# GpSimd's sums of weights on a new timetable, with the order of the first loads, of the pair products and of the parts of x, in a fused attention and matmul-chain kernel

## The reference

```python
scores = q @ k.T / sqrt(64)              # 4 batches, 8 heads, 576 positions, head size 64
scores = where(0 <= i - j < 64, scores, -1e9)
attn = exp(scores - max); attn = attn / (sum(attn) + 1e-9)
x = (attn @ v) as 2304 tokens x 512
x = ((x @ w1) * (x @ w2)) @ w3 @ w_out   # 512 -> 1024 -> 1024 -> 512
h = x @ w_in                             # 512 -> 2048
out = maximum(0.01 * h, h) @ moe2_w_out  # 2048 -> 512, 2304 x 512 out
```

## Time and profile before

| | |
|---|---|
| median of 3 runs | 741.69 us (739.91 to 742.8) |
| profiled execution | 744.82 us, span 742.9 us |
| granted TensorE clock, mean | 0.995 |
| PE (TensorE matmul) busy | 727.1 us, 98% |
| DVE busy | 530.3 us, 71% |
| ACT busy | 417.2 us, 56% |
| POOL busy | 93.3 us, 13%, all before slice 14 of 40 |
| transfers | 181.13 MB, mean 244 GB/s |

### The profile page before, as it was taken

How to read it: one execution, slowest core, us unless ns; L and a number is a source line. 1 busy time by engine, 2 the same in 40 slices (tenths; PEclk the granted TensorE clock), 3 DMA queues, 4 the chain that set the end, 5 groups by cost and what they waited for, 6 DMA issues and landing times.

```text
span 742.9 us, 13803 instructions
## 1 busy us (share of the span) xinstructions
PE 727.1 (98%) x5032; PEld 700.1 (94%) x5032; DVE 530.3 (71%) x833; ACT 417.2 (56%) x889; POOL 93.3 (13%) x122
## 2 busy tenths in 40 slices
PE   8999999799999999999999999999999999999998
PEld 7788898698989999999999999999999999999997
DVE  5988987569657867888867968658788755455552
ACT  5876576536655345656545656456678544444541
POOL 3433574203334000000000000000000000000000
PEclk9999999989999999999999999999999999999999
DMA  9885657645674289988857988988997568777773
GB/s 339 271 292 170 199 184 251 191 155 158 221 241 160 98 271 349 321 276 315 285 195 275 330 293 271 356 303 277 332 375 273 147 163 231 213 211 231 212 199 115
DMA packets 96835, 181.13 MB, mean 244 GB/s; under 512 B 7936, under 2 KB 55680, under 8 KB 96768
## 3 DMA queue, kind: packets, MB, share of 16 engines
q1 hardware_dynamic: 90032, 166.62, 68.4%
q10 hardware_dynamic: 6736, 13.63, 5.0%
HBM read 111.80 MB, written 68.42 MB: 243 GB/s over the span
## 4 chain that ended last, share of the span: by engine, by line
PE 77%; DMA 10%; DVE 6%; issue 2%; SPq 2%; POOL 2%; ACT 1%; DVEq 0%; ACTq 0%
PE acc L402 14%; PE acc L403 14%; PE acc L404 14%; PE ps_pair L403 5%; PE ps_pair L402 5%; PE ps_pair L404 5%; DMA raw_a<-wsum_between 4%; PE ps_more L402 3%; PE ps_values L402 3%; PE ps_more L403 3%; PE ps_values L403 3%; PE ps_more L404 3%; PE ps_values L404 3%; DMA weight_sums<-raw_a 2%; PE ps_values L1672 1%
## 5 line engine op out<-in xcount | busy, mean ns | idle before, releaser
L402 PE MATMUL acc<-parts,weights_a 128*128 128x384 f32 (+1 forms) x320 | 112.2, 351 | 1.9 <-DVE arena L1388 1.3
L402 PE MATMUL acc<-parts,weights_b 128*128 128x384 f32 x320 | 110.3, 345 | 0.9 <-DVE arena L1326 0.5
L404 PE MATMUL acc<-parts,weights_a 128*128 128x384 f32 (+1 forms) x320 | 109.5, 342 | 0.0
L403 PE MATMUL acc<-parts,weights_a 128*128 128x384 f32 (+1 forms) x320 | 109.3, 341 | 0.0
L404 PE MATMUL acc<-parts,weights_b 128*128 128x384 f32 x320 | 108.0, 338 | 0.0
L403 PE MATMUL acc<-parts,weights_b 128*128 128x384 f32 x320 | 108.0, 337 | 0.0
L1457 DVE TENSOR_TENSOR parts<-raw_c,parts 128x768 fp32r<-128x768 f32 x64 | 61.2, 958 | 62.1 <-ACT parts L955 62.0
L955 ACT ACTIVATE parts<-raw_c 128x768 fp32r<-128x768 f32 x64 | 54.0, 846 | 69.6 <-DMA raw_c<-g_between 65.9
L402 PEld LDWEIGHTS acc<-parts,weights_a 128*128 128x128 f32 x320 | 60.1, 188 | 6.8 <-issue 3.1
L402 PEld LDWEIGHTS acc<-parts,weights_b 128*128 128x128 f32 x320 | 60.9, 190 | 2.7 <-issue 0.8
L404 PEld LDWEIGHTS acc<-parts,weights_a 128*128 128x128 f32 x320 | 60.0, 188 | 1.8
(11 more groups left out here) (212 smaller groups left out, 1776.6 us busy)
## 6 DMA issues: line engine op xcount, KB each, us to landing
g_between<-arena SPq DMA_DIRECT2D x75, 384.0 KB, 4.8
raw_c<-g_between SPq DMA_DIRECT2D x64, 384.0 KB, 3.5
arena<-p_between SPq DMA_DIRECT2D x42, 384.0 KB, 5.1
arena<-qk_steps SPq DMA_DIRECT2D x36, 384.0 KB, 5.0
arena<-v_steps SPq DMA_DIRECT2D x36, 256.0 KB, 3.3
p_between<-arena SPq DMA_DIRECT2D x24, 384.0 KB, 5.2
x_between<-arena ACTq DMA_DIRECT2D x21, 384.0 KB, 5.2
arena<-x_between SPq DMA_DIRECT2D x21, 384.0 KB, 5.6
```

What stands on the lines that cost most here:

```text
L402: eng.matmul(out_ap, w_hi, m_hi, start=start, stop=False, skip_group_check=resumed)
L403: eng.matmul(out_ap, w_hi, m_lo, start=False, stop=False, skip_group_check=resumed)
L404: return eng.matmul(out_ap, w_lo, m_hi, start=False, stop=stop, skip_group_check=resumed)
```

## The change

`PRE_SLOT` is new: in the first eight halves twelve slots apart (nine where none of the attention's loads lies), in the last four seven; `load_pre(u+1)` stands four slots after `presums(u)` in place of three. v of steps 0 and 1 is loaded in slot 2, and the first two units of w1 and w2 in slots 1 and 2, in place of ahead of slot 0 and in slot 1. In each round `make_p22` moves up to the second P3 product, and `make_p12` moves behind `make_p21`. The parts of x are split with P3 ahead of P7, and t4 and P4's part later.

```diff
-XS_ORDER = (P2, P1, P5, P6, P7, P3, P4)
+XS_ORDER = (P2, P1, P5, P6, P3, P7, P4)
-PRE_SLOT = (21, 27, 33, 39, 50, 66, 72, 78, 84, 90, 96, 108)
+PRE_SLOT = (24, 36, 48, 57, 69, 81, 93, 105, 115, 122, 129, 136)
+P0_LOAD = {1: 0, 2: 1, 4: 2, 8: 3}
-XS_HI_FIRST = {2: P6, 4: P7, 5: P3, 6: P4}
+XS_HI_FIRST = {2: P6, 3: P3, 4: P7, 7: P4}
-XS_HI_NEXT = {1: P7, 2: P3, 4: P4}
-XS_LO_FIRST = {0: "t2", 1: "t3", 2: P6, 4: "t4", 5: P7, 7: P3, 8: P4}
+XS_HI_NEXT = {1: P3, 2: P7, 7: P4}
+XS_LO_FIRST = {0: "t2", 1: "t3", 2: P6, 4: P3, 5: P7, 6: "t4", 8: P4}
-XS_LO_NEXT = {-1: P6, 0: "t3", 2: P7, 3: "t4", 4: P3, 5: P4}
+XS_LO_NEXT = {-1: P6, 0: "t3", 3: P3, 4: P7, 5: "t4", 8: P4}
@@ SP, before and in the first 16 slots
-            load_v(0)
-            load_fill(0)
-            load_v(1)
-                if k in P0_SUMS and P0_SUMS[k] + 1 < HALF_UNITS:
-                    load_fill(P0_SUMS[k] + 1)
+                if k == 2:
+                    load_v(0)
+                    load_v(1)
+                if k in P0_LOAD:
+                    load_fill(P0_LOAD[k])
@@ SP, stage A/B
-                    if PRE_SLOT[u] + 3 == n and u + 1 < NPRE:
+                    if PRE_SLOT[u] + 4 == n and u + 1 < NPRE:
                         load_pre(u + 1)
@@ DVE, stage A/B
-                if i == P4 and s == 0:
-                    make_p12(r)
+                if i == P3 and s == 1:
                     make_p22(r)
                 if i == P4 and s == 1:
                     make_p21(r)
+                    make_p12(r)
                     p_sum1(r)
```

## The result

The changed kernel takes 745.72 us (median of 6 runs, 743.01 to 746.71), the kernel before 741.24 us in the same comparison (739.91 to 742.8): the ratio is 1.0055, with a 95% interval of 1.0033 to 1.0077. It is slower by half a percent. The forecast was 735.0 us, faster.

A forecast was written before the change was run, and what follows sets the result against it. PE, busy 98%, was taken as the bound, so only its waits and clock counted. 12.0 + 1.6 + 1.2 + 0 - 4.1 - 1.4 - 1.0 = 8.3 us off 744.8 gave 736.5; midway to 733.4, 735.0 (728.5 to 740.5).

The forecast's parts named there:

- Part 1: Halves beside the attention: PE's waits for q, k, v and POOL and the slow clock go; 12.0 us won, at least 8.
- Part 3: Parts of x in round 8: PE's waits for make_c11 and a low part of x go; 1.2 us won (0.5 to 1.2).
- Part 5: Last four halves, without attention: late chain makes PE wait 4.1 us in round 10, and the clock costs 1.4.
- Part 2: Pair products at round ends: PE's waits for make_p21 go, late p12 costs nothing; 1.6 us won (0.6 to 1.6).
- Part 4: First loads, first 20 us: at most 1.0 us won, which can come back; taken as 0, within 1.0 either way.
- Part 6: Denser work: PE asks more of nearly full DVE, so small new waits; 1.0 us lost (0 to 3).
- the slack of ACT: Round 10: spare time before ACT's split of unit 10 (1.9 us) and before the second P7 product (1.4 us).
- the middle cycle: Second of three late store cycles, behind the 1.8 MB of units 8 and 9; expected to wait behind the most bytes.
- the two readings of the 3.1 us: Profiled execution above median: a constant of profiling (733.4 us), or waits or clock not there to win (736.5); middle 735.0 taken.
- The third rival: ACT's split of unit 10, round 10: late chain costs more than all won, some 746 us; chance 0.06.
- the other rivals: Late chain does no harm, 729.5 us, chance 0.22; waits are only moved, 741.0 us, no change, chance 0.12.
- The case on the other side: The third rival: the late chain in round 10 makes the kernel slower, deciding from cycles of 13.2 us; chance 0.06.

The follow-up runs named there:

- half4_earlier: The changed kernel with the fifth half at slot 65 in place of 69: 741.17 us, ratio 0.9996 to the kernel before.
- late_spread: The changed kernel with the last two halves at slots 136 and 150 in place of 129 and 136: 739.19 us, ratio 0.9964 to the kernel before.
- all_three_undone: The changed kernel with first loads in the old order, fifth half at slot 65, last three at 127, 140 and 153: 733.07 us, ratio 0.9901 to the kernel before.
- first_loads_old: The changed kernel with the first loads in the old order, all else as changed: 743.22 us, ratio 1.0025 to the kernel before.
- p12_back: all_three_undone with make_p12 back at the first P4 product and make_p22 left early: 732.71 us, ratio 0.9887 to the kernel before.
- old_pair_order: all_three_undone with both pair products back at the first P4 product: 733.68 us, ratio 0.9902 to the kernel before.
- only_pre: The kernel before with only the new PRE_SLOT and the load four slots behind: 744.35 us, ratio 1.0056.

## Why the prediction was wrong

It had the wrong direction: 745.7 us against 735.0 and a range to 740.5. In the profiled executions the forecast was 8.3 us won and 1.9 were lost, a difference of 10.2. By the matmul starts 5.2 of it are in parts 1 and 3 (13.2 forecast; 9.8 and 1.9 won, 3.7 lost again), 3.4 in part 5, 1.7 in part 2 and 1.3 in part 4; part 6's 1.0 came inside parts 2 and 5, and 0.4 is won behind the last row of the table. Two steps failed above all: the timing of one store in part 1, and the cost of the late chain in part 5.

**Part 1** was right where it looked and failed in one sentence: "A store then comes two slots behind a pair of loads and has three or four slots before the next". That took GpSimd's slot for its time. At slot 69 the half stands behind a normalization that DVE releases some 3 us after the slot's start, and its additions then take 3.0 us. The next load waits 2.6 us for the landing, and the product stores stand in front of v. The waits from 105 to 155 us went as forecast: the same matmul gained 9.8 us there, with the clock, though some 2.5 us of that are a slow clock that the second profile of before does not have. The new wait for v took 3.7 back, and half4_earlier shows its cause. The loads' "two slots later" needs the store's actual time, which the earlier trace rows and the additions behind it would have given.

**Part 5** named the place, the chain and the length of PE's wait: 4.1 us forecast, 4.0 idle in the trace. Its terms were less exact. The cycles had 10.8 us in place of 10.4, but the first store went out at 241.5 while PE was further ahead than assumed, so the load was 9.3 us late and not 7.4; the slack of ACT took more of it, 5.3 and not 3.3. That the wait came out within 0.1 us is therefore luck: the chain was 1.9 us later than forecast and the slack 2.0 larger. Two costs were mis-sized. The clock did fall, 2.7 us in place of 1.4. And the chain held back more than unit 10: units 8 and 9 and round 8's product stores were late too, DVE waited 1.8 us for these products, and its late `make_p21` and `make_c11` put PE back by 1.95 us ahead of round 10's P6, a term that the prediction did not have. Together 8.9 us against 5.5. late_spread shows the wait and its clock, all_three_undone the late sums as well.

The rule of the Trainium skill that a later transfer may complete first ("DMA: Bandwidth & Descriptors", section "Queues, rings and completion order") would have spared the middle cycle. Here the half's load behind the 1.8 MB took 6.4 us and the same load with nothing in front 3.2, by the DMA issues of the changed kernel at 255 and at 267 us:

```profile
raw_a<-w_in_units SPq DMA_DIRECT2D x1, 256.0 KB, 6.4
```
```profile
raw_a<-w_in_units SPq DMA_DIRECT2D x1, 256.0 KB, 3.2
```

The last transfer of unit 9 was issued at 254.83 and landed at 260.9, and the half's landed at 261.7, so it did not pass. Nor did any other: of SP's 459 transfers in this trace 329 share no semaphore with one in flight and have a landing of their own, and none of these landed ahead of an earlier one. The trace doesn't contradict the rule, which says only that nothing forbids it. The middle cycle was the slowest, 12.2 us, as the prediction assumed.

**Part 4** had the chain right (unit, POOL, split, pieces of slot 4) and its size wrong: 0 was taken within 1.0 either way. It cost 1.3 us at slot 4 against the first profile of before and 1.7 in first_loads_old, where the median shows 2.5 with the shorter wait of round 10. The term left out is that POOL waits for the unit ahead of normalization 1, 2.60 us, and that DVE's split then runs beside normalization 1 and takes 1.68 us in place of 0.95.

**Part 2** forecast 1.6 us, and both moves together gave none that could be measured. "The late p12 costs nothing" is the step that failed: no reader of p12 waits, but DVE does the same work later, and `make_c11` of the next round stands behind it. p12_back shows that by taking the waits away. The other move, p22 forward, is worth about 1 us by old_pair_order and p12_back. **Part 3** is unsettled in the times; its two waits went. **Part 6** forecast 1.0 us of new waits for DVE, and PE's waits for line 1327 (2.4 us in four) are of that kind, though they belong to parts 2 and 5.

**The sum** started from an execution that had caught a slow clock. The second profile of before has a span 5.1 us shorter (737.8 and 742.9), 3.2 of it in PE's busy time (723.9 and 727.1), with the clock full. So the difference of an execution to the median is no constant, and of the two readings of the 3.1 us the second was the right one; the prediction went halfway, and 1.5 us of its error are that.

With the measured sizes, the sum from the matmul starts is: 9.8 + 0.5 + 1.9 won, 1.3 + 0.6 + 3.7 + 8.9 lost, -2.3 in all; the span's difference is -1.9. The medians differ by 4.5: the profiled execution of before stands 3.6 us above its median (744.8 and 741.2) and that of after 1.0 (746.7 and 745.7), and 1.9 + 3.6 - 1.0 is 4.5.

The third rival had its place and mechanism right, and its threshold was not reached: it asked for cycles of 13.2 us, with the other parts at full value, and the mean was 10.8. That its "some 746" is near the measured time is luck: it stands for cycles of 14.7 us, and counted from 735.0 like the other rivals it would have been 747.9. The case on the other side came as a sum of this chain, the wait for v and the first loads, none of which outweighs the gain alone.

## What to carry to other kernels

In a list that one engine executes in order, place a waiting instruction by when its condition is met and not by the slot of the work that it waits for: add the lag of the producing engine, and what stands ahead of the work there. Put a store that nobody needs soon behind the loads that somebody does, even if that delays it by ten slots or more. Before work is moved to a quieter stretch, divide that stretch's slot time into the cycle of the chain: here 7 slots of 1.04 us were less than a cycle of 10. And profile the kernel before twice when the effect is half a percent.

## What the runs showed of the hardware

**The clock behind short waits.** TensorE's granted clock fell to 0.50 behind some waits and not behind others of the same size. For three waits in a row at 140 to 149 us: 1.49, 1.70 and 1.36 us in the first profile of before were followed by it; 0.62, 0.66 and 1.36 us in the second were not (clock 1.00 from 146 to 150 us). For the single wait for v at slot 80: 2.4 us in only_pre, 2.6 in the changed kernel and 3.3 in late_spread were followed by it, 2.55 in first_loads_old was not. For the wait for ACT in round 10: 3.2, 3.6, 4.0 and 5.0 us in four kernels were followed by it each time. So for the shorter of these waits one profile does not tell whether they will cost the clock. It cost up to 2.7 us, and the wait of 4.0 us put PE back by 6.9 in all.

**DVE beside GpSimd.** A split of DVE that reads two operands from SBUF took 1.68 us beside GpSimd's normalization and 0.95 in the kernel before at the same place, where none ran beside it. Over the whole trace of the changed kernel that split (128x768, line 1192) took 0.95 to 0.96 us in 20 instructions without GpSimd and 0.95 to 1.80 in 8 with it. DVE's sums with one operand in an accumulator (128x384, lines 1327, 1337 and 1347) took 0.54 to 0.56 us in both cases, 38 of them beside GpSimd.
